# Later expert loads held for the third tile's rows, the gates' one-hots in one place, and ScalarE in place of VectorE for the loop tiles' first inner half

## The reference

```python
logits = einsum('bsd,de->bse', x, w_gate)
local_gate = sigmoid(einsum('bsd,de->bse', x, w_local))
for s in range(S):
    fresh_e = argmax(logits[b, s])
    e = fresh_e if s == 0 or local_gate[b, s] < 0.5 else prev_e
    prev_e = e
    p = softmax(logits[b, s])
    out[b, s] = p[e] * (relu(x[b, s] @ w1[e]) @ w2[e])
```

## Time and profile before

| | us |
|---|---|
| median of 3 runs | 631.39 |
| the profiled execution | 630.64 |
| its span, first to last instruction | 628.6 |
| TensorE busy | 609.6 |
| VectorE busy | 411.8 |
| ScalarE busy | 320.8 |
| GpSimd busy | 161.6 |

### The profile page before, as it was taken

One profiled execution on the slowest core, in us unless ns is written; L12 is line 12 of the kernel. 1 busy time (PEld: TensorE's weight loads), 2 busy tenths in 40 slices (PEclk: granted clock), 3 DMA queues, 4 the chain that ended last, 5 costly groups with the idle time before them and its releaser, 6 DMA issues.

```text
span 628.6 us, 14700 instructions
## 1 busy us (share of the span) xinstructions
PE 609.6 (97%) x4484; PEld 506.7 (81%) x4485; DVE 411.8 (66%) x1166; ACT 320.8 (51%) x697; POOL 161.6 (26%) x239
## 2 busy tenths in 40 slices
PE   7999999999999999999999998979999999999994
PEld 6888888888888888889879876858788888888883
DVE  2777779754888797786889978827726335372621
ACT  4776779677426605723536663537516126351610
POOL 4455445600000000000000202144723512542240
PEclk8999999999999999999999999999999999999998
DMA  8987885002210010000015555577924513672000
GB/s 324 343 281 245 282 283 190 18 2 84 87 48 0 1 61 7 0 33 35 1 50 189 197 218 170 177 288 235 334 99 154 182 44 116 225 249 91 12 28 3
DMA packets 32935, 84.66 MB, mean 135 GB/s; under 512 B 4602, under 2 KB 7418, under 8 KB 32896
## 3 DMA queue, kind: packets, MB, share of 16 engines
q1 hardware_dynamic: 26816, 70.03, 32.3%
q0 software_dynamic: 3200, 8.92, 4.1%
q10 hardware_dynamic: 2880, 5.24, 2.7%
HBM read 76.04 MB, written 9.70 MB: 136 GB/s over the span
## 4 chain that ended last, share of the span: by engine, by line
PE 91%; DVE 3%; DMA 2%; issue 1%; ACT 1%; POOL 1%; ACTq 0%; POOLq 0%; DVEq 0%
PE banks L873 24%; PE banks L875 23%; PE banks L874 23%; PE banks L749 3%; PE banks L1059 3%; PE banks L816 2%; PE banks L825 2%; PE banks L779 2%; PE banks L982 1%; PE banks L763 1%; DMA out_rows<-y,rows_out 1%; PE banks L793 1%; PE banks L789 1%; PE banks L840 1%; PE banks L855 1%
## 5 line engine op out<-in xcount | busy, mean ns | idle before, releaser
L1481 DVE CUSTOM_DVE_ANT_0 product<-x,xT 128x512 f32<-128x512 f32 x120 | 77.9, 687 | 1.3 <-DMA xT<-in_w 1.2
L1791 ACT ACTIVATE prob<-neg,negmax 128x160 f32<-128x160 f32 (+1 forms) x136 | 59.1, 436 | 29.6 <-DVE negmax L1192 19.9
L1769 DVE TENSOR_SCALAR hid<-banks 128x512 f32<-128x512 f32 x34 | 23.5, 691 | 72.6 <-PE banks L875 71.5
L873 PE MATMUL banks<-we_hi,hid_hi 128*128 (+1 forms) x160 | 66.5, 416 | 3.6 <-DVE hid_lo L1594 3.6
L1898 ACT ACTIVATE k_sum<-banks 128x512 f32<-128x512 f32 (+2 forms) x40 | 21.4, 534 | 89.4 <-PE banks L875 84.7
L873 PE MATMUL banks<-we_hi,xg_hi 128*128 (+1 forms) x160 | 65.3, 408 | 0.8 <-issue 0.8
L875 PE MATMUL banks<-we_hi,xg_lo 128*128 (+1 forms) x160 | 63.2, 395 | 0.0
L874 PE MATMUL banks<-we_lo,xg_hi 128*128 (+1 forms) x160 | 63.1, 394 | 0.0
L875 PE MATMUL banks<-we_hi,hid_lo 128*128 (+1 forms) x160 | 62.6, 391 | 0.0
L874 PE MATMUL banks<-we_lo,hid_hi 128*128 (+1 forms) x160 | 62.5, 391 | 0.0
L873 PE MATMUL banks<-mix_hi,wk_hi 128*128 128x512 f32 (+2 forms) x160 | 57.4, 358 | 0.2 <-POOL wr_lo L578 0.2
(11 more groups left out here) (293 smaller groups left out, 1486.0 us busy)
## 6 DMA issues: line engine op xcount, KB each, us to landing
xT<-in_w_e SPq DMA_DIRECT2D x36, 512.0 KB, 4.6
raw_end<-in_w_e SPq DMA_DIRECT2D x36, 512.0 KB, 4.8
qk<-in_qk_t SPq DMA_DIRECT2D x32, 448.0 KB, 6.0
vw<-in_v_t SPq DMA_DIRECT2D x32, 256.0 KB, 5.2
w_raw<-in_w_mix ACTq DMA_DIRECT2D x20, 256.0 KB, 4.3
x_rows<-x SPq DMA_DIRECT2D x17, 256.0 KB, 2.0
xT<-in_w SPq DMA_DIRECT2D x8, 256.0 KB, 3.4
vz<-in_v_z SPq DMA_DIRECT2D x8, 128.0 KB, 3.5
```

Of the source, the lines that this page charges most:

```text
L873: pe.matmul(dst, left[0], right[0], start=first, stop=False)
L1481: dve.tensor_tensor_reduce(product[:, k % 2, :], x2[:, t, :], w9(e), 1.0, 0.0, ALU.mult, ALU.add, dot[:, t % 2, e:e + 1]).then_inc(dotted, 1)
L1769: dve.tensor_scalar(hid[:, D * h:D * (h + 1)], ps_h[:, h, :], 0.0, None, ALU.max).then_inc(hid_ready, 1)
L1791: act.activation(prob[:, t % 2, c], neg[:, c], ACT.Exp, scale=-1.0, bias=negmax[:, t % 2, k:k + 1], accum_out=rsum[:, t % 2, k:k + 1]).the ...
```

## The change

SyncE waits for `xg_turned` 3, the transposes of tile 2's rows, ahead of its loop over `r`. On VectorE, the remainder of part 3 of round 1 moves behind `rest_of_rows(2)`; all six products for the gates stand behind `rest_of_hidden(2, 0)`; the two reductions come ahead of `rest_of_rows(3)` and part 7. On ScalarE, ahead of the loop, the wait for `y_summed` 3 is gone and `relu_hidden(2, 0)` stands first, the roundings of round 2 stand each one step later, and parts 2 and 3 come between `round_hidden(2, 1)` and the wait for `gates_ready`. In the loop the ReLU of half 0 is ScalarE's, behind the first two roundings of the next weights; VectorE keeps half 1. `relu_hidden` of ScalarE is the function at L1942 to L1946, unchanged.

```diff
--- before.py
+++ after.py
@@ -530,6 +530,7 @@
                 store(first_tile(GROUPS - 1) + t, t)
             for j in range(2, PARTS):
                 load_next_part(j)
+            sp.wait_ge(xg_turned, 3)
             with sp.Fori(2, E + 1) as r:
                 for j in range(PARTS):
 
@@ -1680,9 +1681,10 @@
             after(own)
             picked = done(dve.tensor_tensor(work[:], lexp[:], work[:], ALU.mult))
             rest_of_hidden(1, 1)
-            for j in range(1, PARTS // 2):
+            for j in range(1, PARTS // 2 - 1):
                 rest_of_part(1, slice(1, 2), j)
             rest_of_rows(2)
+            rest_of_part(1, slice(1, 2), PARTS // 2 - 1)
 
 
             end = ntile[0:1, 1, :].unsqueeze(1).broadcast_to([1, LATER, E])
@@ -1730,23 +1732,22 @@
 
             for j in range(PARTS // 2, VPARTS):
                 rest_of_part(1, slice(1, 2), j)
+            rest_of_hidden(2, 0)
             after(gates_split)
             for k in range(3):
                 dve.tensor_tensor(by_gate_early[:, :, k, :], by_tile_early[:, :, 0, :], by_token(gate_part[:, k, 0:NA], EARLY),
                                   ALU.mult)
-            dve.tensor_tensor(by_gate[:, :, 0, :], by_tile[:, :, 0, :], by_token(gate_part[:, 0, :], LATER), ALU.mult)
-            rest_of_hidden(2, 0)
-            for k in range(1, 3):
+            for k in range(3):
                 ins = dve.tensor_tensor(by_gate[:, :, k, :], by_tile[:, :, 0, :], by_token(gate_part[:, k, :], LATER), ALU.mult)
             ins.then_inc(gate_onehots_ready, 1)
             rest_of_part(1, slice(1, 2), VPARTS)
             rest_of_hidden(2, 1)
-            rest_of_rows(3)
             dve.wait_ge(gates_summed, 1)
-            rest_of_part(1, slice(1, 2), VPARTS + 1)
             dve.tensor_reduce(slot_gate[:, 0:EARLY], ps_chain_odd[:, 0:3 * EARLY].rearrange("p (k m) -> p m k", k=3), AX.X, ALU.add)
             dve.tensor_reduce(slot_gate[:, EARLY:MT], ps_chain[:, 0:3 * LATER].rearrange("p (k m) -> p m k", k=3), AX.X,
                               ALU.add).then_inc(gates_ready, 1)
+            rest_of_rows(3)
+            rest_of_part(1, slice(1, 2), VPARTS + 1)
             for j in range(VPARTS):
                 rest_of_part(2, slice(0, 1), j)
 
@@ -1762,17 +1763,14 @@
                             for j in parts:
                                 rest_of_part(following, bass.ds(following % 2, 1), j)
 
-                    def relu_hidden(h):
-
-                        dve.wait_ge(hid_summed, 2 * i + h + 1)
-                        dve.wait_ge(hid_lo_ready, 2 * i + h + 1)
-                        dve.tensor_scalar(hid[:, D * h:D * (h + 1)], ps_h[:, h, :], 0.0, None,
-                                          ALU.max).then_inc(hid_ready, 1)
-
-                    relu_hidden(0)
                     weights_of_next(range(0, 1))
                     rest_of_hidden(i, 0)
-                    relu_hidden(1)
+
+                    dve.wait_ge(hid_ready, 2 * i + 3)
+                    dve.sem_inc(stepped, 1)
+                    dve.wait_ge(hid_summed, 2 * i + 2)
+                    dve.wait_ge(hid_lo_ready, 2 * i + 2)
+                    dve.tensor_scalar(hid[:, D:2 * D], ps_h[:, 1, :], 0.0, None, ALU.max).then_inc(hid_ready, 1)
                     weights_of_next(range(1, 2))
                     with dve.If(i + 1 < tiles):
                         rest_of_rows(i + 1)
@@ -1979,12 +1977,10 @@
             copy_y(1)
 
 
-            act.wait_ge(y_summed, 3)
+            relu_hidden(2, 0)
             rounded_weights(2, slice(0, 1), range(0, 1))
-            relu_hidden(2, 0)
+            round_hidden(2, 0)
             rounded_weights(2, slice(0, 1), range(1, 2))
-            round_hidden(2, 0)
-            rounded_weights(2, slice(0, 1), range(2, 3))
 
             def weigh_y(b):
                 act.wait_ge(y_copied, b + 1)
@@ -1993,10 +1989,11 @@
             relu_hidden(2, 1)
             round_rows(3)
             round_hidden(2, 1)
+            rounded_weights(2, slice(0, 1), range(2, 4))
             act.wait_ge(gates_ready, 1)
             weigh_y(0)
             weigh_y(1)
-            rounded_weights(2, slice(0, 1), range(3, 6))
+            rounded_weights(2, slice(0, 1), range(4, 6))
 
             def finish_y(i, b, before_it):
                 act.wait_ge(y_stored[b], 16 * before_it)
@@ -2018,6 +2015,7 @@
                             act.wait_ge(y_summed, i + 1)
                             act.sem_inc(stepped, 1)
                             rounded_weights(after, bass.ds(after % 2, 1), range(0, 2))
+                        relu_hidden(i, 0)
                         for h in range(2):
                             round_hidden(i, h)
                             if h == 0:
```

## The result

The changed kernel takes 637.74 us (median of 6 runs, 636.08 to 638.17); the kernel before, timed beside it, 631.12 (629.20 to 631.49). The ratio is 1.0108, 95% interval 1.0091 to 1.0125: 6.6 us slower. The forecast was 631.1 with a range to 632.8. The profiled execution took 638.17, with a span of 636.2; its times run 0.36 us later than before's from early on, which is to be taken off in comparisons. One of the seven executions of a later kernel ("ReLU back, VectorE yields") took 2113.52 us; its median of 628.12 is taken over all seven (627.99 without that one), its ratio over the other six.

What follows compares the result with a forecast made beforehand. TensorE, busy 97% of the span, was taken as the bound. Outputs 4.0 us earlier, 1.7 lost to the clock and 2.0 in the loop gave -0.3, hence 631.1 us against a 631.39 median; range 628.0 to 632.8.

Steps and rivals of the forecast that it cites:

- those that it named for tiles 2 and 3: Tile 2's row transposes right behind the matmul, clock 1.00 after; one pause before tile 3's hid transposes, ReLU behind scatter's landing.
- SyncE's wait, and the clock of tile 2: Tile 2: holding loads lets the gather land earlier, saving a 1.04 us pause; 2.4 GHz stays, saving 1.68 us.
- VectorE's new order is hidden: Ahead of the loop: VectorE's moved remainders and one-hot products finish before TensorE needs them, with 0.3 to 0.5 us spare.
- Its landing decides the rest ... I take 5.8: Tile 0's scatter, started at 401.2, lands 5.8 us later at 407.0; bounds 2.6 and 7.4.
- ScalarE's ReLU at tile 3: Tile 3: ReLU behind finish_y(2) and two roundings; one 3.1 us pause replaces 0.81 and 3.41, outputs 4.0 us earlier.
- The rival that has the scatter hold the ReLU: Tile 3: landing takes 7.4 us as now and delays the transposes too; +1.3 us, 632.7 us, chance 0.15.
- The clock falls in tile 3's pause: Tile 3: the wholly idle 3.1 us pause brings a clock fall costing 1.7 us; bounds 0 and 1.7.
- The ReLU in the loop: Loop: six tiles make TensorE wait for ScalarE's ReLU behind two roundings, costing 1.97 us; bounds 0 and 3.6.

Runs made afterwards that it cites:

- ReLU back, VectorE yields: Changed kernel with the loop's first ReLU back on VectorE, and VectorE waiting before round 2's remainders until GpSimd issued tile 0's scatter: 628.12 us, ratio 0.9967.
- order only: Changed kernel without SyncE's wait and with VectorE's ReLU in the loop, leaving only VectorE's and ScalarE's new order ahead of it: 636.43 us, ratio 1.0082.
- loop's ReLU only: Kernel before with the loop's first ReLU on ScalarE, nothing else: 632.76 us, ratio 1.0043.
- ReLU back, VectorE yields, no wait: Changed kernel without SyncE's wait, loop's first ReLU back on VectorE, VectorE waiting before round 2's remainders for the issue of tile 0's scatter: 628.61 us, ratio 0.9959.
- VectorE yields: Changed kernel with VectorE waiting, ahead of its six remainders of round 2, until GpSimd has issued tile 0's scatter: 628.17 us, ratio 0.9969.
- SyncE's wait only: Kernel before with SyncE's new wait for xg_turned 3 ahead of the loop over r, nothing else: 630.83 us, ratio 1.0003.
- ReLU back: Changed kernel with the loop's first ReLU given back to VectorE, the rest of the change kept: 634.49 us, ratio 1.0060.

## Why the prediction was wrong

Of the signs that the prediction named as its being wrong none came (the gather as late as now, a landing under 5 us, no waits in the loop), and those that it named for tiles 2 and 3 did. It had no sign for a landing later than its bounds, and that is what came.

1. **SyncE's wait, and the clock of tile 2**: right in size, 2.7 us (1.10 and 1.58, forecast as 1.04 and 1.68). The 1.10 is the wait's. The 1.58 is not shown to be: the three other profiled kernels without the wait (order only; loop's ReLU only; ReLU back, VectorE yields, no wait) have the gather's pause (0.75, 0.58 and 0.81) and the one behind it (0.76), and yet keep 2.4 GHz in tile 2, so that it was in part luck that the profile of before had a fall to give back. This may be why the median moves less than the profile.
2. **VectorE's new order is hidden**: nearly right. Gates, one-hots and y's weighing came to within 0.2 us of the forecast times once the offset is off. Part VPARTS + 1 came in time for the outputs that use it (forecast 401.0, ended at 401.03 with the offset off, used from 401.4), as forecast, but not for what stands behind them: tile 3's first matmul starts 2.65 us behind its end both in before (402.94 to 405.59) and in after (401.39 to 404.05), and in after TensorE's own work no longer fills that stretch. The prediction had no term for it; it is the pause of 0.78, where before had none, 0.8 us. What fills the 2.65 us is open.
3. **"Its landing decides the rest ... I take 5.8"**: this is the step that failed. The bounds, 2.6 and 7.4, were rows of two different scatters, whose issue takes 0.99 to 1.48 (all 20 of before), and the step carried that issue along unsaid. The runs show what it took: 13.4, of which 7.5 are the issue, held by VectorE's row. The order caused it ("order only" has it, 7.49). By what in the order is argued, not tested: the reductions moved up, the scatter with them, and ScalarE had by then rounded part 3 too, so that ready remainders stood behind the running one at every boundary. In before part 3 was still being rounded when the scatter got in. Once the hold is away the landing is 4.8 (VectorE yields), better than the 5.8.
4. **ScalarE's ReLU at tile 3**: the place was right, one pause ahead of the transposes, and its size went with step 3: 9.9 in place of 3.1. The rival that has the scatter hold the ReLU named the mechanism that decided, but priced the landing with before's 7.4, +1.3 in all; with 13.4, six us more, it gives +7.3, and the profiled execution lost 7.5.
5. **The clock falls in tile 3's pause**: right, 1.6 us. From the transposes to `finish_y(3)` pass 10.51 us, against 12.28 - 3.41 = 8.87 before.
6. **The ReLU in the loop**: 1.97 forecast, 1.61 measured. The six tiles lose 0.23, 0.57, 0.16, 0.16, 0.19 and 0.51, 1.82 together against 1.97; tile 6, behind the second of them, wins 0.28 back.

Together: -2.7 + 0.8 + 5.9 (pauses of 9.92 where there were 0.66 and 3.41) + 1.6 = 5.6, the 5.6 at `finish_y(3)`, and 1.6 in the loop.

The Trainium skill bears on this order from two sides. "SBUF — State Buffer", section "Who interferes with whom": VectorE shares a pair of SBUF ports with GpSimd as an exclusive lock, and an operation of VectorE with two SBUF inputs contends with a GpSimd operation that reads SBUF. The remainder has two such inputs, the scatter's row numbers lie in SBUF, and the trace agrees that GpSimd is held (7.51 us against 1.00). That it is by this read is not shown. The same section adds that a probe saw `tensor_tensor` not stall descriptor generation, the work of such an issue, and infers that it needs only the pair's write interface; here a row of just that operation held the issue, and the measurement decides. The page speaks of a lock for one instruction; here the hold lasts over six, and by one remainder alone it would be at most 1.14 us.

## What to carry to other kernels

Before a scatter or gather of GpSimd is moved, look at what VectorE runs at its new time, as well as at what the DMA queues do: its issue is work of GpSimd, and a long row of VectorE's operations with both inputs in SBUF can hold it to the row's end. Which rows do is known only for the cases below. Where a tight transfer has to go out, let VectorE wait for it once ahead of the row, or break the row with waits; here 1.5 us of VectorE's idle time bought 8.8 to 9.6. And follow a gain to the end of the kernel: of the 2.7 us that "SyncE's wait only" had at tile 2, 0.4 were left at the last `finish_y`, since the clock fell behind a later pause.

## What the runs showed of the hardware

- The hold was seen only where further remainders stood ready behind the running one, and that alone isn't enough for it. A scatter that came 0.27 to 1.03 us into a remainder was held over the whole row (after and six kernels with its order). It got in at the first boundary where the next but one was not yet ready (before and the two kernels with its order, 0.64 in), where each waited for the last (two kernels, 0.28 in), and where the row had started behind a wait (five kernels, 0.88 in). Why the last lets GpSimd in is open.
- VectorE wasn't slowed while it held GpSimd (1.14 us a remainder). The other way round it was: with GpSimd's own subtractions started between, two remainders took 4.5 us in place of 2.35 (three kernels).
- VectorE's ReLU right behind the row, which reads the accumulator, did not prolong the hold: in "ReLU back" it starts at 407.78 and the issue still ends at 408.76, 0.90 behind the last remainder.
- The granted clock didn't follow the pause's length alone: no fall behind pauses of 3.41 (before) and 1.94, a fall behind 1.99, 2.10, 3.63 and 4.30. Nor is it the same in every execution of one kernel: the twelve of "VectorE yields" have a mean granted clock between 0.990 and 0.997 and took 626.32 to 631.38 us. What decides was not found.
